# Two of a pair's 15 products exchange places, and the two chain banks exchange roles in every second pair

## The chip, the cores and the metric

One core of a Trainium2 chip runs the kernel. The metric is the device time of one execution in microseconds (us). An engine or queue is named as the profile names it: PE is TensorE's matmul, PEld its weight load, DVE is VectorE, ACT is ScalarE, POOL is GpSimd, SP is SyncE.

## The reference

A linear-attention recurrence over 768 steps for 2 x 8 heads of 48 gives x with 1536 rows and 384 columns. It then goes through four dense experts and a last gated layer:

```
p = domain_probs / (domain_probs.sum(-1) + 1e-9)
for e in range(4):                                   # w1[e] 384 x 1024, w2[e] 1024 x 384
    out += p[:, e:e+1] * (maximum(x @ w1[e], 0) @ w2[e])
h = out @ w_in                                       # 384 x 2048
y = (h * sigmoid(1.702 * h)) @ w_out                 # 2048 x 384
```

All of it is float32; the kernel splits every operand in a high and a low part and does three matmuls (high-high, high-low, low-high) where one product stands.

## The kernel before, in words

**Stages.** The attention and the first expert run first, mixed, up to about 150 us. Expert 1 to 3 and the gated layer then run as 20 "pairs" (numbered from 0): a pair is two tiles of 128 hidden columns each. Pair 12 (PLAIN), where the gated layer begins, is done in the plain way; the other 19 have both tiles against the 1536 rows, cut in three blocks of 512 rows, in the Strassen manner: 15 products on sums of weights and sums of rows in the place of 18.

**A product** (`product`, line 1946 in the profile) is three matmuls of 128x512 into one PSUM bank. The table PRODUCT (line 124) has its 15 rows in order: weight sum, rows, bank, whether it begins a new sum in its bank or goes on adding to what the bank holds, and then what is done with the bank: "copy" (ACT, `take`, line 1230) or "add" (DVE, `join`, lines 1570 and 1572) into result o, with a sign. The two banks, LEFT = 5 and RIGHT = 6, are the chain banks. A product waits until the copy or join of the product before it in the same bank has read the bank. In pair 0 some products use bank 3 or 4 instead (FIRST_BANKS, line 394): products 0, 12 and 13 use bank 3.

**A result** is one of six tiles: o = 3f + n, hidden tile f and row block n. The last product that goes into a result (LAST_OF) settles when it is complete, and DONE is the order in which the six get complete: place 0 is the first. By places, DVE gates the tile (`tile_gate`, line 1603), ACT copies its high part (`tile_high`, line 1248), and DVE takes its low part (`tile_low`, line 1613).

**A group** (`group`, line 1993) is six matmuls: the second weights of both hidden tiles against the tiles of row block n, three with f = 0 and three with f = 1, for output chunk k. A pair has nine, n in the order 1, 2, 0. The half for f waits until the low part of that tile is there. The groups of pair q stand on PE between the products of pair q + 1. A group's result is in bank 0 or 1, or by turns in banks 3 and 4 (SHARED); DVE adds it to the accumulator (`leave`, line 1585 or 1590). The very first group goes to bank 3, and so waits until pair 0's last use of bank 3 is over.

**The order** of each engine's work is a list made by `pairs`, and then, for some stretches, written out by hand (WRITTEN): p is a product, g a group, t a copy, j a join, m a gate, h a high part, l a low part, e a group's leaving; the number before the point is the pair. Each engine runs its list in that order. The stretch of DVE's list around the end of pair 0 reads

```
"... j0.10 j0.11 j0.12 m0.2 l0.0 j0.13 l0.1 l0.2 m0.3 j0.14 m0.4 j1.1 l0.3 m0.5 e0.1.0 j1.3 ..."
```

and PE's order there is p0.12, p0.13, p0.14, p1.0, g0.1.0 (the first group: pair 0, n = 1, k = 0), p1.1, p1.2, g0.1.1. Products of other pairs stand between groups, as in `p1.13 p1.14 g0.0.1 p2.0 g0.0.2 p2.1 p2.2`.

Of the kernel before, what the change touches and what calls it, by code (L numbers as in the profile page):

```python
# [122 lines left out]
LEFT, RIGHT = 5, 6  # L123
PRODUCT = (
    (2, (1, 0), LEFT, True, "copy", 0, 1),
    (10, (0, 0), LEFT, True, "add", 0, 1),
    (0, (1, 1), RIGHT, True, "copy", 1, 1),
    (12, 8, LEFT, False, "add", 1, -1),
    (9, 13, RIGHT, True, "copy", 4, 1),
    (7, 3, LEFT, False, "copy", 2, 1),  # L130
    (11, (2, 1), RIGHT, False, "add", 1, 1),
    (4, (0, 2), LEFT, False, "copy", 5, 1),
# [2 lines left out]
    (1, 4, LEFT, False, "add", 4, -1),  # L135
    (14, 10, RIGHT, False, "add", 5, -1),
    (6, (2, 2), LEFT, True, "add", 5, -1),
    (3, 1, LEFT, False, "add", 3, -1),
    (5, (1, 2), RIGHT, False, "add", 2, -1),
)  # L140

SUM_HOME = {13: 0, 8: 1, 14: 2, 3: 3, 9: 4, 1: 5, 10: (0, 1), 4: (2, 0)}
# [66 lines left out]
ADDED = [i for i, row in enumerate(PRODUCT) if row[4] == "add"]  # L209
# [5 lines left out]
def build(nc, rkT, rkvN, wu_rows, u_rows, weights, out):  # L215
    p_dram = nc.dram_tensor("p_normalised", [E, N], F32, kind="Internal").ap()
    ctx = ExitStack()
    with ctx:
# [10 lines left out]
        sem = {}  # L229
# [161 lines left out]

        OUT_SETS = ((7, 6, 5), (0, 1, 2))
        KEPT, SHARED, OVER = (0, 1), (3, 4), (2, 7)
        FIRST_BANKS = {0: SHARED[0], 2: SHARED[1], 12: SHARED[0], 13: SHARED[0]}
        PLAIN_BANKS, FIRST_OVER = (*OVER, LEFT, RIGHT), (OVER[1], SHARED[1], OVER[0], *KEPT, OVER[1])

        def out_tile(n, k):
# [125 lines left out]
        def kept_last(q):  # L523

            return q in (MOE_PAIRS - 1, ALL_PAIRS - 1)

        def kept_first(q):

            return q in (0, MOE_PAIRS)

        def kept(n, k):

            return n == 0 and k < len(KEPT)
# [6 lines left out]
        def wait_left(engine, q, n, k):  # L540

            if q == PLAIN:
                engine.wait_ge(sem["fresh"], THROUGH.index((n, k)) + 1)
            else:
                engine.wait_ge(sem["evac"], LEAVES[q, n, k] + 1)
# [5 lines left out]
        def place_of(q, f, n):  # L551

            return 2 * ROUND.index(n) + f if q == PLAIN else DONE.index(3 * f + n)
# [16 lines left out]

        def bank_of(q, i):

            return FIRST_BANKS.get(i, PRODUCT[i][2]) if q == 0 else PRODUCT[i][2]

        def result_of(q, pos):

# [12 lines left out]
        def shared_number(q, n, k):  # L589

            return len(THROUGH) * q + THROUGH.index((n, k))

        def shared_at(number):

            return (number // len(THROUGH), *THROUGH[number % len(THROUGH)])

        def shared_bank(q, n, k):

            return SHARED[shared_number(q, n, k) % len(SHARED)]
# [482 lines left out]
        def _(act):  # L1082
# [136 lines left out]
            def take(q, i):  # L1219

                _, _, _, _, _, o, sign = PRODUCT[i]
                number = t_number(q, o)
                act.wait_ge(sem["prod"], PRODS[q] + i + 1)
                if number >= T_RING:
                    act.wait_ge(sem["added"], t_before(number))
                    if q == 1:
                        act.wait_ge(sem["l2"], STEPS)
                elif t_tile(number) is t_of[number]:
                    act.wait_ge(sem["l2"], STEPS - 2)
                act.activation(t_tile(number), bank[:, bank_of(q, i), :], ACT.Copy, scale=float(sign)).then_inc(sem["copied"], 1)  # L1230
# [62 lines left out]
        def _(dve):  # L1293
# [252 lines left out]
            def join(q, i):  # L1546

                _, _, _, _, _, o, sign = PRODUCT[i]
                at = bank_of(q, i)
                t = t_tile(t_number(q, o))  # L1550
                before = [x for x in ADDED if x < i and PRODUCT[x][5] == o]
                dve.wait_ge(sem["prod"], PRODS[q] + i + 1)
                if before:
                    dve.wait_ge(sem["added"], JOINED[q] + ADDED.index(before[-1]) + 1)
                else:
                    dve.wait_ge(sem["copied"], TAKEN[q] + COPY_OF.index(o) + 1)
                new = t
                if LAST_OF[o] == i:
                    pos = DONE.index(o)
                    new = over_bank(q, pos)  # L1560
                    if q:
                        dve.wait_ge(sem["tlo"], 6 * q + pos - len(OVER) + 1)
                    elif pos == 1:
                        dve.wait_ge(sem["copied"], COPIED.index(2) + 1)
                    elif 1 < pos < 5:
                        dve.wait_ge(sem["ev1"], KT * len(SPANS))
                    elif pos == 5:
                        dve.wait_ge(sem["tlo"], 1)
                if sign > 0:
                    dve.tensor_tensor(new, bank[:, at, :], t, ALU.add).then_inc(sem["added"], 1)  # L1570
                else:
                    dve.scalar_tensor_tensor(new, bank[:, at, :], -1.0, t, ALU.mult, ALU.add).then_inc(sem["added"], 1)  # L1572
# [73 lines left out]
        def _(pe):  # L1646
# [275 lines left out]
            def product(q, i):  # L1922

                weight, rows, _, begins, _, _, _ = PRODUCT[i]
                at = bank_of(q, i)
                piece = next(n for n, (first, last) in enumerate(PIECES) if first <= weight < last)
                pe.wait_ge(sem["alo"], PARTS_W[q] + piece + 1)
                if q in (0, PLAIN + 1) and type(rows) is int:
                    pe.wait_ge(sem["slo"], len(SUM_ORDER) * (q > 0) + SUM_ORDER.index(rows) + 1)
                if q == PLAIN + 1 and i in (0, 2):  # L1930
                    pe.wait_ge(sem["tlo"], 6 * PLAIN + (3 if at == LEFT else 4))
                earlier = [x for x in range(i) if bank_of(q, x) == at]
                if earlier:
                    x, before = earlier[-1], q
                elif q and q != PLAIN + 1:
                    x, before = max(x for x in range(PRODUCTS) if bank_of(q - 1, x) == at), q - 1
                else:
                    x = None
                    if at in HID:
                        pe.wait_ge(sem["hlo"], STEPS - 1 + HID.index(at))  # L1940
                if x in COPIED:
                    pe.wait_ge(sem["copied"], TAKEN[before] + COPIED.index(x) + 1)
                elif x in ADDED:
                    pe.wait_ge(sem["added"], JOINED[before] + ADDED.index(x) + 1)
                for n, (a, c) in enumerate(PASSES):
                    last = pe.matmul(bank[:, at, :], a_parts[a][:, q % 2, weight * P:(weight + 1) * P], rows_of(ss[c], xs[c], rows),  # L1946
                                     start=(begins and n == 0), stop=(n == 2), skip_group_check=True)
                last.then_inc(sem["prod"], 1)
# [20 lines left out]
            def group(q, n, k):  # L1969

                begins, ends = (kept_first(q), kept_last(q)) if kept(n, k) else (True, True)
                if kept(n, k):
                    at = KEPT[k]
                    if q == 0:
                        pe.wait_ge(sem["ev1"], KT * len(SPANS))
                        pe.wait_ge(sem["tlo"], FIRST_OVER.index(at) + 1)
                    elif begins:
                        pe.wait_ge(sem["evac"], LEAVES[q - 1, n, k] + 1)
                else:
                    at = shared_bank(q, n, k)  # L1980
                    number = shared_number(q, n, k)
                    if number >= len(SHARED):
                        wait_left(pe, *shared_at(number - len(SHARED)))
                    elif number == 0:
                        pe.wait_ge(sem["added"], ADDED.index(13) + 1)
                    else:
                        pe.wait_ge(sem["tlo"], FIRST_OVER.index(at) + 1)
                pe.wait_ge(sem["vlo"], q + 1)
                for f in range(2):
                    number = 6 * q + place_of(q, f, n)  # L1990
                    pe.wait_ge(sem["tlo"], number + 1)
                    for i, (a, c) in enumerate(PASSES):
                        last = pe.matmul(bank[:, at, :], v_parts[a][q % 2][:, f * DM + k * P:f * DM + (k + 1) * P], tiles[c][number % H_RING],  # L1993
                                         start=(begins and f == 0 and i == 0), stop=(ends and f == 1 and i == 2))
                last.then_inc(sem["grp"], 1)
# [74 lines left out]
```

## Time and profile before

| | |
|---|---|
| median of 3 runs | 609.37 us (609.34 to 609.57) |
| the profiled execution | 609.61 us, span 607.6 us |
| PE busy | 598.9 us, 99% |
| DVE / ACT / POOL busy | 461.4 / 295.3 / 307.1 us |
| granted TensorE clock | 1.00 |

The time of an execution is that of its span and some 2 us around it. A row of a timeline gives start, duration, engine, line, operation, tiles out and in, and count; in brackets stands how long the engine had been idle and what released it. Matmuls are pipelined, so the duration of one (0.39 us) is longer than the distance between two starts (0.227 us); stalls are read from the starts.

### The profile page before, as it was taken

Reading aid. Unit: us, or ns where it says so; the run is one execution under the profiler, and the core shown is the slowest. Engines: PE = TensorE matmul, PEld = TensorE weight load, DVE = VectorE, ACT = ScalarE, POOL = GpSimd, SP = SyncE. Lnnn points to the kernel's source line nnn. Section 1 sums busy time; section 2 is a strip of 40 time slices with the busy share of each in tenths; the row PEclk is TensorE's granted clock in tenths of the full one; section 3 lists DMA queues with packets and bytes.
Section 4 is the critical chain, followed back from the end, with each engine's and each line's share of the span. In section 5 each row is a group of like instructions: output and inputs, shape, how many; then the busy total and the mean of one; then the engine's idle time right before and its main releaser. Section 6 shows DMA issues by size and latency. Waiting matters only on the chain.

```text
span 607.6 us, 10788 instructions
## 1 busy us (share of the span) xinstructions
PE 598.9 (99%) x3709; PEld 496.4 (82%) x3709; DVE 461.4 (76%) x752; ACT 295.3 (49%) x585; POOL 307.1 (51%) x369
## 2 busy tenths in 40 slices
PE   8999999989999999999999999999999999999997
PEld 5999988867688888888888888888887888888886
DVE  7888563454888877877877877788787887877895
ACT  4754533143544445345345335335776566556540
POOL 5654310599566455455446446326776745544200
PEclk9999999999999999999999999999999999999999
DMA  8766430001211110210010110100101110100004
GB/s 328 276 231 208 133 125 2 3 2 50 81 52 53 52 54 17 88 53 28 26 53 26 28 53 26 53 26 2 31 23 52 53 53 26 28 26 1 1 0 156
DMA packets 18171, 39.14 MB, mean 64 GB/s; under 512 B 1984, under 2 KB 9792, under 8 KB 18112
## 3 DMA queue, kind: packets, MB, share of 16 engines
q1 hardware_dynamic: 18112, 38.40, 18.8%
q8 instruction: 32, 0.52, 0.4%
q14 instruction: 27, 0.22, 0.1%
HBM read 36.01 MB, written 2.38 MB: 63 GB/s over the span
## 4 chain that ended last, share of the span: by engine, by line
PE 94%; DVE 2%; issue 1%; POOL 1%; DMA 1%; ACT 0%; SPq 0%; DVEq 0%; POOLq 0%; ACTq 0%
PE bank L1993 40%; PE bank L1946 32%; PE bank L1687 7%; PE bank L1712 7%; PE bank L1965 2%; PE bank L1746 2%; PE bank L1790 1%; PE bank L1793 1%; PE bank L1765 1%; PE bank L1780 1%; DMA rk_in<-rk_t 1%; PE bank L1783 0%; DVE s_lo L1538 0%; DVE acc L1623 0%; DVE bank L1572 0%
## 5 line engine op out<-in xcount | busy, mean ns | idle before, releaser
L1993 PE MATMUL bank<-w_lo,w_hi 128*128 128x512 f32 x729 | 186.1, 389 | 0.0
L1020 POOL TENSOR_TENSOR a_lo<-staging,a_hi 128x512 fp32r<-128x512 f32 (+3 forms) x96 | 97.7, 1026 | 146.9 <-ACT a_hi L1208 135.6
L1993 PEld LDWEIGHTS bank<-w_lo,w_hi 128*128 128x128 f32 x729 | 136.7, 188 | 29.0 <-DVE w_lo L1613 0.4
L1230 ACT ACTIVATE t_most<-bank 128x512 f32<-128x512 f32 x110 | 65.7, 598 | 55.7 <-PE bank L1946 54.9
L1993 PE MATMUL bank<-w_hi 128*128 128x512 f32 x351 | 91.8, 389 | 0.0
L1248 ACT ACTIVATE w_lo<-bank 128x512 fp32r<-128x512 f32 x81 | 48.0, 598 | 84.9 <-DVE bank L1603 52.9
L1585 DVE TENSOR_TENSOR acc<-bank,acc 128x512 f32<-128x512 f32 x86 | 58.7, 685 | 25.8 <-PE bank L1993 25.8
L1993 PEld LDWEIGHTS bank<-w_hi 128*128 128x128 f32 x351 | 65.9, 188 | 13.7
L1572 DVE SCALAR_TENSOR_TENSOR bank<-bank,t_most 128x512 f32<-128x512 f32 x92 | 63.9, 695 | 14.9 <-PE bank L1946 12.4
L1946 PE MATMUL bank<-x_hi,a_hi 128*128 128x512 f32 x171 | 66.6, 390 | 0.1
L1946 PE MATMUL bank<-x_lo,a_hi 128*128 128x512 f32 x171 | 66.5, 389 | 0.0
L1946 PE MATMUL bank<-x_hi,a_lo 128*128 128x512 f32 x171 | 66.5, 389 | 0.0
L1025 POOL TENSOR_TENSOR w_hi<-staging,w_hi 128x768 fp32r<-128x768 f32 x20 | 37.0, 1851 | 45.5 <-ACT w_hi L1217 45.5
L1613 DVE TENSOR_TENSOR w_lo<-bank,w_lo 128x512 fp32r<-128x512 f32 x81 | 55.3, 684 | 3.5 <-ACT w_lo L1248 1.2
L1208 ACT ACTIVATE a_hi<-staging 128x512 fp32r<-128x512 f32 (+2 forms) x95 | 48.0, 521 | 9.7 <-POOL staging L1061 5.7
L1946 PE MATMUL bank<-s_hi,a_hi 128*128 128x512 f32 x114 | 44.7, 392 | 1.6 <-DVE bank L1572 1.2
L1946 PE MATMUL bank<-s_lo,a_hi 128*128 128x512 f32 x114 | 44.4, 389 | 0.0
L1946 PE MATMUL bank<-s_hi,a_lo 128*128 128x512 f32 x114 | 44.4, 389 | 0.0
L1248 ACT ACTIVATE w_hi<-bank 128x512 fp32r<-128x512 f32 x39 | 23.3, 598 | 41.2 <-DVE bank L1603 26.6
L1109 ACT ACTIVATE h_hi<-bank 128x256 fp32r<-128x256 f32 (+1 forms) x32 | 15.6, 487 | 55.7 <-PE bank L1687 55.7
L1370 DVE SCALAR_TENSOR_TENSOR h_lo<-bank,h_hi 128x256 fp32r<-128x256 f32 (+1 forms) x32 | 17.6, 551 | 32.7 <-ACT h_hi L1109 32.6
L1946 PEld LDWEIGHTS bank<-x_hi,a_hi 128*128 128x128 f32 x171 | 32.1, 188 | 7.4 <-issue 0.5
(179 smaller groups left out, 1152.2 us busy)
## 6 DMA issues: line engine op xcount, KB each, us to landing
staging<-weights SPq DMA_DIRECT2D x40, 384.0 KB, 3.6
rkv_in<-rkv_n SPq DMA_DIRECT2D x10, 640.0 KB, 5.5
rk_in<-rk_t SPq DMA_DIRECT2D x12, 512.0 KB, 5.2
staging<-weights SPq DMA_DIRECT2D x4, 768.0 KB, 8.9
out<-acc SPq DMA_DIRECT2D x9, 256.0 KB, 2.0
p_bc<-p_normalised SPq DMA_DIRECT2D x2, 768.0 KB, 4.1
staging<-p_normalised SPq DMA_DIRECT2D x2, 768.0 KB, 5.6
rkv_in<-rkv_n SPq DMA_DIRECT2D x2, 448.0 KB, 5.8
```

What stands on the lines that cost most here:

```text
L1020: pool.tensor_tensor(new, src, high.bitcast(F32), ALU.subtract).then_inc(sem["alo"], 1)
L1025: pool.tensor_tensor(v_lo[q % 2], second_raw[q % 2], v_hi[q % 2].bitcast(F32), ALU.subtract).then_inc(sem["vlo"], 1)
L1208: act.activation(a_hi[:, q % 2, first * P:last * P].rearrange("p (i n) -> p i n", n=P), src, ACT.Copy).then_inc(sem["ahi"], 1)
L1230: act.activation(t_tile(number), bank[:, bank_of(q, i), :], ACT.Copy, scale=float(sign)).then_inc(sem["copied"], 1)
L1248: act.activation(tile_hi[number % H_RING], over_bank(q, pos), ACT.Copy).then_inc(sem["thi"], 1)
L1572: dve.scalar_tensor_tensor(new, bank[:, at, :], -1.0, t, ALU.mult, ALU.add).then_inc(sem["added"], 1)
L1585: dve.tensor_tensor(acc[:, k, cols], src, acc[:, k, cols], ALU.add).then_inc(sem["evac"], 1)
L1613: dve.tensor_tensor(tile_lo[number % H_RING], over_bank(q, pos), tile_hi[number % H_RING].bitcast(F32), ALU.subtract).then_inc(sem["tlo"], 1)
L1687: last = pe.matmul(bank[:, HID[j % 2], 0:tokens.stop - tokens.start], w[:, k, :], xs[c][:, k, tokens], start=(n == 0), stop=(n == 3 * KT - 1))
L1712: last = pe.matmul(out_tile(n, k), w[:, k * P:(k + 1) * P], hs[c][:, slot, 0:size],   start=(first and i == 0 and not (n < SMALLS and k == ...
L1946: last = pe.matmul(bank[:, at, :], a_parts[a][:, q % 2, weight * P:(weight + 1) * P], rows_of(ss[c], xs[c], rows), start=(begins and n == ...
L1993: last = pe.matmul(bank[:, at, :], v_parts[a][q % 2][:, f * DM + k * P:f * DM + (k + 1) * P], tiles[c][number % H_RING], start=(begins and ...
```

## The change

In PRODUCT the last two rows change places: product 13 is now the one in bank RIGHT that completes result 2, and product 14 the one in bank LEFT that completes result 3. DONE was 1, 0, 4, 5, 3, 2 and is now 1, 0, 4, 5, 2, 3. In pair 0, product 14 instead of 13 goes to bank 3, and the first group waits for the join of product 14 instead of 13. In pairs with an even number above 0, LEFT and RIGHT are exchanged. The lists of orders are as they were; they name products and results by their number and place.

```
@@ PRODUCT
     (6, (2, 2), LEFT, True, "add", 5, -1),
+    (5, (1, 2), RIGHT, False, "add", 2, -1),
     (3, 1, LEFT, False, "add", 3, -1),
-    (5, (1, 2), RIGHT, False, "add", 2, -1),
 )
@@ build
-        FIRST_BANKS = {0: SHARED[0], 2: SHARED[1], 12: SHARED[0], 13: SHARED[0]}
+        FIRST_BANKS = {0: SHARED[0], 2: SHARED[1], 12: SHARED[0], 14: SHARED[0]}
@@ bank_of
-            return FIRST_BANKS.get(i, PRODUCT[i][2]) if q == 0 else PRODUCT[i][2]
+            if q == 0:
+                return FIRST_BANKS.get(i, PRODUCT[i][2])
+
+            return LEFT + RIGHT - PRODUCT[i][2] if q % 2 == 0 else PRODUCT[i][2]
@@ group
                     elif number == 0:
-                        pe.wait_ge(sem["added"], ADDED.index(13) + 1)
+                        pe.wait_ge(sem["added"], ADDED.index(14) + 1)
```

## Rows read from the trace of the kernel before

**Rows 1.** The page: span, and PE's share of it.

```profile
span 607.6 us, 10788 instructions
...
PE 598.9 (99%) x3709; PEld 496.4 (82%) x3709; DVE 461.4 (76%) x752; ACT 295.3 (49%) x585; POOL 307.1 (51%) x369
```

**Rows 2.** Waits of PE on DVE at products: us in total, times, longest.

```profile
PE bank L1946 <- DVE bank L1572: 1.2, 2, 1.0
PE bank L1946 <- DVE t_rest L1570: 0.2, 1, 0.2
PE bank L1946 <- DVE t_most L1570: 0.2, 1, 0.2
```

**Rows 3.** The chain that ended last, its last three pieces (start, us, what).

```profile
588.07 16.33 PE bank L1993 x72
604.40 0.02 issue
604.43 0.69 DVE acc L1590
```

**Rows 4.** Timeline of PE from product 11 of pair 0 on.

```profile
159.10 0.39 PE L1946 MATMUL bank<-x_hi,a_lo 128*128 128x512 f32 x1
159.33 0.40 PE L1946 MATMUL bank<-x_hi,a_hi 128*128 128x512 f32 x1
...
161.15 0.47 PE L1946 MATMUL bank<-s_hi,a_hi 128*128 128x512 f32 x1 [0.98 <-DVE bank L1572]
...
161.92 0.39 PE L1946 MATMUL bank<-x_hi,a_hi 128*128 128x512 f32 x1
...
162.60 0.39 PE L1946 MATMUL bank<-x_hi,a_hi 128*128 128x512 f32 x1
...
163.28 1.74 PE L1993 MATMUL bank<-w_lo,w_hi 128*128 128x512 f32 x6
164.86 0.40 PE L1946 MATMUL bank<-x_hi,a_hi 128*128 128x512 f32 x1
```

**Rows 5.** Timeline of DVE in the same stretch.

```profile
159.53 0.69 DVE L1572 SCALAR_TENSOR_TENSOR part<-bank,part 128x512 f32<-128x512 f32 x1 [0.32 <-PE bank L1946]
160.31 0.70 DVE L1572 SCALAR_TENSOR_TENSOR bank<-bank,part 128x512 f32<-128x512 f32 x1
160.91 0.69 DVE L1603 SCALAR_TENSOR_TENSOR bank<-bank,staging 128x512 f32<-128x512 f32 x1
161.51 0.68 DVE L1613 TENSOR_TENSOR w_lo<-bank,w_lo 128x512 fp32r<-128x512 f32 x1
162.12 0.70 DVE L1572 SCALAR_TENSOR_TENSOR bank<-bank,t_most 128x512 f32<-128x512 f32 x1
162.72 1.28 DVE L1613 TENSOR_TENSOR w_lo<-bank,w_lo 128x512 fp32r<-128x512 f32 x2
163.92 0.69 DVE L1603 SCALAR_TENSOR_TENSOR bank<-bank,staging 128x512 f32<-128x512 f32 x1
164.52 0.69 DVE L1572 SCALAR_TENSOR_TENSOR bank<-bank,part 128x512 f32<-128x512 f32 x1
165.12 0.69 DVE L1603 SCALAR_TENSOR_TENSOR bank<-bank,staging 128x512 f32<-128x512 f32 x1
165.75 0.69 DVE L1570 TENSOR_TENSOR t_most<-bank,t_most 128x512 f32<-128x512 f32 x1
...
168.47 0.69 DVE L1572 SCALAR_TENSOR_TENSOR t_most<-bank,t_most 128x512 f32<-128x512 f32 x1 [0.24 <-PE bank L1946]
```

**Rows 6.** Weight loads of PE at the stalled product and in the first group.

```profile
161.12 0.19 PEld L1946 LDWEIGHTS bank<-s_hi,a_hi 128*128 128x128 f32 x1 [1.37 <-issue]
...
164.06 0.53 PEld L1993 LDWEIGHTS bank<-w_lo,w_hi 128*128 128x128 f32 x3 [0.36 <-DVE w_lo L1613]
```

**Rows 7.** Busy time by stretch: PE, PEld, DVE, ACT, POOL, granted clock, DMA share.

```profile
166.00:604.40 438.40, 438.19 (x1931) 361.77 (x1929) 352.25 (x547) 221.13 (x400) 219.94 (x272) 1.00 0.12 38
```

**Rows 8.** Timeline of PE at the start of the program.

```profile
1.39 3.59 PE L1650 MATMUL bank<-part 128*128 128x512 bf16 x8 [1.39 <-POOL part L846]
4.81 1.09 PE L1658 MATMUL bank<-ident,w_rev 128*128 128x128 f32 x4
5.69 0.86 PE L1650 MATMUL bank<-part 128*128 128x512 bf16 x2
6.63 1.16 PE L1746 MATMUL bank<-q_r_mid,q_k_mid 48*128 48x128 f32 x16
```

## The prediction

> **What bounds the kernel now.** I read the page first: PE is busy for 598.9 of 607.6 us [rows 1], so only what makes PE wait, or takes waits from it, can move the time. A busy PE may still hide small losses, because its matmul ends are modelled, so I turned to the waits. In the whole of the pairs PE waits for DVE at four places, 1.6 us in sum, and the longest is one of 1.0 us [rows 2]. From 166.00 to 604.40 us PE is busy for 438.19 of 438.40 us [rows 7]. The chain that ended last is groups without a break, then one DVE add [rows 3]. Its 72 matmuls give the pace of a PE that never waits: 16.33 / 72 = 0.2268 us from start to start, so a product costs 0.68 us and a group 1.36 us.
>
> How much could be hidden between? From the start of the first group at 163.28 [rows 4] to the end of the last matmul at 604.40 [rows 3] the program has 20 x 9 groups of 6, 18 pairs of 15 products of 3 less the 3 matmuls of the product that stands ahead of that group, and 6 x 9 plain ones: 1080 + 807 + 54 = 1941 matmuls. A matmul's end is 0.39 us after its start, so from first start to where the next would start there are 604.40 - 0.39 + 0.23 - 163.28 = 440.96 us; 1941 x 0.2268 = 440.2. About 0.7 us is lost in all of this, and two waits that can be named (0.22 us in the first group, below, and one of rows 2 with its restart, some 0.3) are most of it. Everything that the change loosens in pairs 1 to 19 is worth at most this 0.7 us.
>
> **Pairs 1 to 19: each wait that changes.** Product 13 now waits for the join of product 11 instead of that of 12, and product 14 for that of 12 instead of 11. The join of 12 was needed by product 13 and is now needed by the one behind it: looser by 0.68 us. Products 0 and 2 of the next pair waited for the joins of 13 and 14, in that order, and still do, because the exchange of LEFT and RIGHT in even pairs follows the exchange of the rows; without it product 0 would wait for the join of 14. The tiles: row block 2 needed places 3 and 5, now 3 and 4; row block 0 needed 1 and 4, now 1 and 5. Its groups are the last three of a pair, so the last tile has three groups (4.1 us) more. The copy into result 3's buffer in the next pair waits one join longer, but it is the sixth copy there, nine products on. A tile's high part waits for the last group of its ring slot's reader: at one place that is now the last group of the pair two before, which runs as the pair begins, while the high parts come in its second half. The same operations run in the same order on every engine, so there is no new instruction and no DMA is moved. Since PE hardly waits there, I cost all this at nothing. What covers it is PE's own queue, which is full; the end behind the last matmul [rows 3] is the same as well. The bound is a gain of 0.7 us.
>
> **The end of pair 0: this is where it is decided.** Here there are no groups between the products, and each wait shows. The rows read like this [rows 4]: product 11's last matmul starts at 159.10, product 12 at 159.33. Product 13 could start at 159.33 + 0.68 = 160.01, but it is in bank 3 like product 12 and waits for join 12, which DVE has from 160.31 to 161.01 [rows 5]; it starts at 161.15, 0.14 us behind the join's end. Product 14 starts at 161.92, product 0 of pair 1 at 162.60, the first group at 163.28, product 1 of pair 1 at 164.86. The group takes 164.86 - 163.28 = 1.58 us and not 1.36: its second half waits for the low part of place 2, the second of the two operations that end at 162.72 + 1.28 = 164.00, and its weights load at 164.06 [rows 6].
>
> Now with the change:
> - Product 13 goes to RIGHT and waits for join 11, which ends at 159.53 + 0.69 = 160.22. It starts at 160.22 + 0.14 = 160.36 instead of 161.15. It takes 0.77 us, as after every restart here (161.92 - 161.15), to 161.13.
> - Product 14 goes to bank 3 and waits for join 12: 161.01 + 0.14 = 161.15. Product 0 of pair 1 follows at 161.83, and PE is ready for the first group at 161.83 + 0.68 = 162.51. So far 0.77 us are won.
> - The first group uses bank 3 and must now wait for join 14. What is DVE doing? Its list has join 13, two low parts, a gate, and then join 14. In rows 5 those are 162.12, 162.72 (two), 163.92 and 164.52, and from 160.31 to 166.4 they follow each other without a pause, 0.60 us apart: DVE is backed up, so an earlier product doesn't bring any of them forward. Nothing ahead of them changes: joins 11 and 12 read products that start when they did, and the exchange of results changes only which buffer joins 13 and 14 read. Join 14 ends at 164.52 + 0.69 = 165.21.
> - The group starts at 165.21 + 0.14 = 165.35 instead of 163.28: 2.07 us later. The low part of place 2 has been there since 164.00, so the wait in the middle is gone. It takes 1.36 + 0.09 for the restart = 1.45 us, and product 1 of pair 1 starts at 166.80 instead of 164.86: **1.94 us later**.
> - Who is late next? Behind the waiting group on PE stands product 1 of pair 1, and join 1 of pair 1 waits for that. It started at 165.75 [rows 5], when DVE got to it; now DVE gets to it at the same time and waits until about 167.7, and what follows in its list (a low part, a gate, the leaving of the first group) is late by the same 1.9 us. They serve groups that are as late. DVE's first idle moment in before, 0.24 us at 168.47, shows that it follows PE again by then, so the ratio between the two is as before.
> - Is the delay made good later? PE has no pause that it could give up but the 0.5 us that remain in the bound above, and the operations behind these pauses are late together with PE. So it goes through to the end.
>
> Sum: 609.61 + 1.94 = 611.55 us for an execution like the profiled one; the median of before is 0.24 us lower: 609.37 + 1.94 = **611.3 us**, 0.32% slower.
>
> The unknown sizes: the restart and the semaphore (0.09 and 0.14 us) are each seen more than once, and an error is under 0.1. The bound of what the loosened waits give back is 0.7 us, so 610.6 at the low end. At the high end one more DVE operation (0.60 us) could come ahead of join 14, or the restarted group could need another restart: 612.0. I take the middle because each row of the sum is seen in the trace itself.
>
> **The rivals.**
>
> *The first group isn't held (no change).* If join 14 came straight after join 13 or the gate and low parts were quicker, so that it ended before 162.4 us, PE would run into the group at 162.51. Its second half would still wait for the low part of place 2, which DVE has at 164.00, and product 1 of pair 1 would start at 164.86 as before: 609.4 us. Against it speaks that DVE's order is fixed and rows 5 show it without a gap. I give this 7%.
>
> *The stall at product 13 is won and kept (faster).* This is the same with the low part of place 2 early as well: PE keeps the 0.77 us and the 0.22 us in the group: 609.37 - 0.99 = 608.4 us. It is decided by one thing, whether DVE has finished both the low part of place 2 and join 14 by some 163.1 us; in rows 5 they end at 164.00 and 165.21. 3%; even then the gain is 0.16%, under what can be told from no change.
>
> *The clock falls during the pause (slower still).* PE will be idle from the end of product 0 of pair 1 (161.83 + 2 x 0.23 + 0.39 = 162.7) to 165.35, 2.7 us. The waits of before in rows 2 are 1.0 us at most, so no row shows what a pause of 2.7 us does to the clock; the granted clock is 1.00 after all of them [rows 7]. What a low clock costs is seen at the start: eight matmuls of 512 columns start in 4.81 - 1.39 = 3.42 us, 0.43 us apiece, which is the pace of 1.2 GHz (although the clock's column says 1.00 there), and the slow stretch is over by 6.63 us [rows 8]. If PE went back to that state and needed as long to leave it, half of 6.63 - 1.39 = 5.2 us would be lost, 2.6 us: 613.9 us. The Trainium skill, "TensorE: Matmul & The Clock Gate", section "HAM oscillation — how this bites in real kernels", says that gaps in PE's work make the gate throttle it again, so that the work behind a gap starts at half rate. By that rule a single gap could bring this rival about; the trace neither shows nor excludes it. Since PE works without a pause both before and after this one gap, I give it 5%.
>
> **How the numbers follow.** The forecast has 85% (611.3 us), no change 7%, the kept gain 3%, the clock 5%. The measurement can tell about 0.2%, 1.2 us, from no change; the forecast's 1.94 us is above this, and its low end of 610.6 is right at it. Slower by over 0.2%: 85 + 5 less 2 for the forecast's low edge = 88%. Within 0.2%: 7 + 2 and most of the kept gain's 3, 10%. Faster: 2%, for a gain in the later pairs on top of the kept one. The range is that of the forecast, 610.6 to 612.0, wider by 0.2 us on each side for the distance between a profile and a median: 610.4 to 612.2 us. That leaves out the rivals, 15%.
>
> **What would show it.** In the trace after: product 13 of pair 0 starts near 160.4 and not 161.15, and the wait of 1.0 us at it shrinks to about 0.3. A new wait of PE (or of its weight load) on line 1993 for DVE line 1572 stands at about 162.5 to 165.3, 2.7 us long, and it is the longest in the pairs. On DVE the join at 162.12 reads the buffer `part` and the one at 164.52 `t_most`, the other way round than before. DVE gets an idle spell of nearly 2 us ahead of the join at about 167.7. All starts behind that are 1.9 us later, and the pace stays at 0.2268. I am wrong if DVE reaches join 14 sooner than 164.5, if new or vanished waits stand in pairs 1 to 19, or if starts are 0.43 us apart after the pause.

## The result, and the profile after

| | before | after |
|---|---|---|
| median | 609.47 us (609.34 to 609.91, 6 runs) | 613.0 us (611.47 to 613.35, 6 runs) |
| ratio | | 1.005, 95% interval 1.004 to 1.006 |
| the profiled execution | 609.61 us, span 607.6 us | 613.08 us, span 611.0 us |

The kernel became 0.5% slower. The forecast was 611.3 us, in a range of 610.4 to 612.2 us. The six executions took 611.47, 612.07, 612.92, 613.08, 613.12 and 613.35 us: two lie in the range, one of them at the forecast, and four lie above it. That spread, 1.9 us, is the first thing to see. The kernel before has 0.6 us here and 1.1 to 1.5 us in the larger batches below, where one of its 67 executions, at 1548.99 us, is left out; so the spread alone proves little, and the clock has to be read with it.

The page gives the new wait in its costliest group (before, then after). In the kernel before, groups had no idle time ahead of them:

```profile
L1993 PE MATMUL bank<-w_lo,w_hi 128*128 128x512 f32 x729 | 186.1, 389 | 0.0
```

```profile
L1996 PE MATMUL bank<-w_lo,w_hi 128*128 128x512 f32 x729 | 186.7, 391 | 2.5 <-DVE bank L1575 2.5
```

(All lines of the kernel after are 3 higher: products 1949, groups 1996, joins 1573 and 1575, gates 1606, low parts 1616.) The timeline of PE at the end of pair 0, against [rows 4]:

```profile
159.76 0.39 PE L1949 MATMUL bank<-x_hi,a_lo 128*128 128x512 f32 x1
160.33 0.47 PE L1949 MATMUL bank<-x_hi,a_hi 128*128 128x512 f32 x1 [0.18 <-DVE part L1575]
...
161.12 0.47 PE L1949 MATMUL bank<-s_hi,a_hi 128*128 128x512 f32 x1
...
161.89 0.39 PE L1949 MATMUL bank<-x_hi,a_hi 128*128 128x512 f32 x1
...
165.21 2.26 PE L1996 MATMUL bank<-w_lo,w_hi 128*128 128x512 f32 x6 [2.46 <-DVE bank L1575]
167.27 0.63 PE L1949 MATMUL bank<-x_hi,a_hi 128*128 128x512 f32 x1
167.70 0.63 PE L1949 MATMUL bank<-x_lo,a_hi 128*128 128x512 f32 x1
168.12 0.63 PE L1949 MATMUL bank<-x_hi,a_lo 128*128 128x512 f32 x1
...
169.66 1.55 PE L1996 MATMUL bank<-w_lo,w_hi 128*128 128x512 f32 x6
```

and that of DVE, against [rows 5]:

```profile
162.08 0.69 DVE L1575 SCALAR_TENSOR_TENSOR bank<-bank,part 128x512 f32<-128x512 f32 x1
162.68 1.28 DVE L1616 TENSOR_TENSOR w_lo<-bank,w_lo 128x512 fp32r<-128x512 f32 x2
163.87 0.69 DVE L1606 SCALAR_TENSOR_TENSOR bank<-bank,staging 128x512 f32<-128x512 f32 x1
164.47 0.69 DVE L1575 SCALAR_TENSOR_TENSOR bank<-bank,t_most 128x512 f32<-128x512 f32 x1
165.07 0.69 DVE L1606 SCALAR_TENSOR_TENSOR bank<-bank,staging 128x512 f32<-128x512 f32 x1
168.79 0.69 DVE L1573 TENSOR_TENSOR t_most<-bank,t_most 128x512 f32<-128x512 f32 x1 [3.03 <-PE bank L1949]
```

What to see. Up to the first group all is as forecast: product 13 at 160.33, product 14 at 161.12 without a stall, product 0 of pair 1 at 161.89, join 14 on `t_most` at 164.47 to 165.16, the group at 165.21. Then the forecast fails: matmuls start 0.43 us apart (167.27, 167.70, 168.12) instead of 0.227. The windows show why; the clock column stands ahead of the DMA share:

```profile
162.00:164.00 2.00, 0.75 (x4) 0.27 (x2) 2.00 (x5) 1.42 (x3) 0.00 (x0) 1.00 0.00 0
164.00:166.00 2.00, 0.79 (x3) 0.67 (x4) 1.76 (x3) 1.22 (x4) 1.18 (x2) 1.00 0.01 4
166.00:168.00 2.00, 2.00 (x6) 1.60 (x5) 0.00 (x0) 0.00 (x0) 1.93 (x3) 0.51 0.31 66
168.00:170.00 2.00, 2.00 (x7) 1.53 (x7) 1.21 (x3) 0.14 (x1) 2.00 (x3) 0.64 0.89 320
170.00:172.00 2.00, 2.00 (x11) 1.63 (x10) 1.35 (x4) 1.46 (x3) 1.33 (x2) 1.00 0.02 8
```

Behind the pause the granted clock is 0.51, that is 1.2 GHz of the two levels 1.2 and 2.4, and in the next 2 us it comes back. Six matmuls stand in a window that has ten or eleven at 2.4 GHz. Half-microsecond windows place the two edges:

```profile
165.50:166.00 0.50, 0.50 (x3) 0.39 (x3) 0.26 (x1) 0.00 (x0) 0.43 (x1) 1.00 0.00 0
166.00:166.50 0.50, 0.50 (x3) 0.39 (x2) 0.00 (x0) 0.00 (x0) 0.43 (x1) 0.52 0.00 0
169.00:169.50 0.50, 0.50 (x3) 0.40 (x2) 0.50 (x2) 0.00 (x0) 0.50 (x1) 0.57 1.07 426
169.50:170.00 0.50, 0.50 (x4) 0.41 (x3) 0.50 (x2) 0.14 (x1) 0.50 (x2) 1.00 0.60 240
```

The column still reads 1.00 all through the pause. It falls at about 166.0, some 0.8 us after the group has started, and is back at about 169.4. The group's own length says the same: six matmuls at 0.43 us would take 2.56 us, at 0.227 us 1.36 us, and it takes 167.27 - 165.21 = 2.06 us, so its first matmuls ran at full pace.

Measured from product 12's last matmul (159.79 before, 159.76 after), the second group starts 166.23 - 159.79 = 6.44 us later in the kernel before and 169.66 - 159.76 = 9.90 us later in this one: 3.46 us lost at one place. The two parts can be told apart here. The group starts 5.45 us behind that matmul instead of 3.49, 1.96 us late; had it then taken the forecast 1.45 us instead of the 1.58 us of before, the loss would be 1.83 us, and the other 1.63 us are the slow matmuls. Nothing is lost or won behind it. The chain after has the same last stretch, 72 matmuls in 16.33 us as in [rows 3], and ends 3.46 us later:

```profile
591.53 16.33 PE bank L1996 x72
607.86 0.02 issue
607.88 0.69 DVE acc L1593
```

But those windows show a second thing that happens at the same time: the DMA share is 0.89 where the matmuls are slow. The traces already speak against the transfers as the cause. The matmuls are slow from 166.0 us on, while the share is still 0.00, and the kernel before has the same burst under matmuls at full clock:

```profile
168.00:170.00 2.00, 2.00 (x10) 1.65 (x10) 1.75 (x4) 1.97 (x4) 2.00 (x2) 1.00 0.91 305
```

Experiment 1 tries it in the changed kernel.

### The profile page after: what moved, and what is told of

Its sections match the earlier page's. It is cut to its first block, busy times and chain, and to the rows that moved or that the text cites. A ratio compares the mean times of both kernels' runs of the same rounds, so it can differ in the third digit from the quotient of the medians.

```text
span 611.0 us, 10788 instructions
## 1 busy us (share of the span) xinstructions
PE 600.4 (98%) x3709; PEld 497.7 (81%) x3709; DVE 461.3 (76%) x752; ACT 295.3 (48%) x585; POOL 307.4 (50%) x369
## 4 chain that ended last, share of the span: by engine, by line
PE 93%; DVE 3%; issue 2%; POOL 1%; DMA 0%; ACT 0%; DVEq 0%; POOLq 0%; ACTq 0%
PE bank L1996 40%; PE bank L1949 31%; PE bank L1690 7%; PE bank L1715 7%; PE bank L1968 2%; PE bank L1749 2%; PE bank L1793 1%; PE bank L1796 1%; PE bank L1783 1%; PE bank L1768 1%; PE bank L1786 0%; DMA wu_sb<-wu_rows 0%; DVE s_lo L1541 0%; DVE bank L1575 0%; DVE w_pow L1301 0%
```

## The experiments

They were run in three batches, each on another chip and each beside the kernel before on the same chip. Experiments 1 to 4 are the first batch and 5a, 6, 7a and 7b the second, both with a median of 609.66 us for the kernel before; 5b, 5c and 5d are the third, with 609.58 us. The mean granted clock of an execution is 1.000 or 0.999 where nothing fell (the kernel before has both). Theory A: the wait for join 14 costs 1.9 us, and the pause that it makes lets the clock fall, which costs the rest. Theory B: the rest comes from the transfers. Theory C: it comes from the later pairs.

**1. The pause filled with work** (added to the kernel after).

```
                     product(q, *rest)
+                    if (q, *rest) == (1, 0):
+                        pe.wait_ge(sem["added"], ADDED.index(13) + 1)
+                        for _ in range(9):
+                            pe.matmul(bank[:, RIGHT, :], a_parts[0][:, 1, 2 * P:3 * P], xs[0][:, 1, 0:NB], start=True, stop=True, ...)
```

> The changed kernel with nine extra matmuls, whose result nobody reads, in bank 6 between product 0 of pair 1 and the first group. Theory A (the wait for join 14 costs 1.9 us, and the rest of the loss is TensorE's clock, which fell because of the pause): the group starts when it did, near 165.2, the pause shrinks from 2.6 to under 0.5 us, the granted clock stays at 1.00, and the time is 611.3 us in every execution, without the spread of 611.5 to 613.4. Theory B (the rest of the loss comes from elsewhere, as a burst of DMA that slows the matmuls behind the group): matmuls behind the group still start 0.43 us apart for some 4 us, and the time stays near 613.0.

Measured: 611.53 us (611.27 to 611.83, 5 runs), ratio 1.0034 (1.0021 to 1.0047). PE's timeline and its windows:

```profile
162.72 2.32 PE L2008 MATMUL bank<-x_hi,a_hi 128*128 128x512 f32 x9
165.11 1.66 PE L1996 MATMUL bank<-w_lo,w_hi 128*128 128x512 f32 x6
166.60 0.39 PE L1949 MATMUL bank<-x_hi,a_hi 128*128 128x512 f32 x1
```

```profile
165.20:167.00 1.80, 1.80 (x8) 1.49 (x9) 0.45 (x1) 0.08 (x1) 1.50 (x3) 1.00 0.00 0
167.00:169.00 2.00, 2.00 (x10) 1.65 (x10) 1.51 (x3) 0.83 (x2) 2.00 (x3) 1.00 0.83 252
```

Nine useless matmuls make the kernel some 1.5 us faster (611.53 against 613.0 us, and against 612.93 us in experiment 4 of the same batch). The group starts no sooner (165.11), but the clock stays at 1.00, the spread is 0.6 us, and the same burst of transfers (share 0.83) passes under matmuls at full pace. Theory B is out.

**2. The wait alone**, in the kernel before: `ADDED.index(13) + 1` becomes `ADDED.index(14) + 1`, and nothing else changes.

> The kernel before with one wait lengthened: the first group waits for the join of product 14 instead of 13. No row of PRODUCT and no bank is exchanged. Theory A: join 14 ends at 165.2 as in both kernels, so the group starts at 165.35 and product 1 of pair 1 at 166.8, 1.94 us late; the pause in front of the group is 2.07 less 0.2 us, a fifth shorter than the 2.6 us of the changed kernel, so the clock falls as often or less often: 611.4 us where it does not fall, up to 613.4 where it does. Theory C (the later pairs' exchange is what costs the rest): 611.4 us in every execution, granted clock 1.00.

Measured: 611.33, 611.35, 612.18, 613.22 and 613.24 us, ratio 1.004 (1.0027 to 1.0053). PE waits 1.8 us at the first group, and in the profiled execution (613.24 us) the windows 165.20 to 167.00 and 167.00 to 169.00 have a clock of 0.73 and 0.50. The lengthened wait alone brings both parts of the loss.

**3. The change in pairs 1 to 19 alone.** The table, the order of completion and the banks depend on the pair (cut, against the kernel after):

```
+EXCHANGED = (*PRODUCT[:13], PRODUCT[14], PRODUCT[13])
+def rows_in(q):
+    return EXCHANGED if q == 0 else PRODUCT
...
-        FIRST_BANKS = {0: SHARED[0], 2: SHARED[1], 12: SHARED[0], 14: SHARED[0]}
+        FIRST_BANKS = {0: SHARED[0], 2: SHARED[1], 12: SHARED[0], 13: SHARED[0]}
```

and the first group waits for join 13.

> The change in pairs 1 to 19 alone: pair 0 has its rows, its banks and its wait as before. Theory A: the looser waits of the later pairs give nothing and cost nothing: 609.4 us, within 0.3, PE starts its first group at 163.3 with the 1.0 us stall at product 13 back. Theory C: the later pairs cost 1.7 us: 611.1 us. The bound of a gain is 0.7 us: 608.8.

Measured: 609.38 us (609.14 to 610.5, 11 runs), ratio 1.0000 (0.9991 to 1.0009). PE's waits in the pairs are those of before, the 1.0 us at product 13 among them. Theory C is out, and the looser waits of 18 pairs give nothing that can be told (the interval is 0.5 us to either side).

**4. The change in pair 0 alone**: `EXCHANGED` and `PRODUCT` the other way round, no exchange of banks in even pairs.

> The change in pair 0 alone: the later pairs keep their rows and banks. Theory A: the whole of the loss, with its spread: 611.4 to 613.4 us, median 613.0, group at 165.2, clock down for 4 us behind it in most executions. Theory C: 611.3 us, no spread.

Measured: 612.93 us (611.68 to 613.8, 6 runs), ratio 1.0051 (1.0039 to 1.0063): two executions at 611.7, four from 612.8 to 613.8. It is the whole of the change's effect, with its spread. That this run would have no fall under theory C was badly put; the pause is in pair 0 under any theory, so it tells only where the loss is.

**5. How the clock depends on the pause.** Join 14 is moved in DVE's list, in the kernel after; the rest of the list is as it was.

```
 after:  ... j0.13 l0.1 l0.2 m0.3 j0.14 m0.4 j1.1 l0.3 m0.5 ...
 5a:     ... j0.13 j0.14 l0.1 l0.2 m0.3 m0.4 j1.1 l0.3 m0.5 ...
 5b:     ... j0.13 l0.1 j0.14 l0.2 m0.3 m0.4 j1.1 l0.3 m0.5 ...
 5c:     ... j0.13 l0.1 l0.2 j0.14 m0.3 m0.4 j1.1 l0.3 m0.5 ...
 5d:     ... j0.13 l0.1 l0.2 m0.3 m0.4 l0.3 j0.14 j1.1 m0.5 ...
```

5a: 

> The changed kernel with join 14 of pair 0 moved on DVE to stand right behind join 13, ahead of two low parts and a gate. Theory A: join 14 ends near 163.4 instead of 165.2, the group starts at 163.5 after a pause of 0.9 us, its second half waits for the low part of place 2, now 0.6 us later (164.6), and product 1 of pair 1 starts near 165.4: 0.6 us later than in the kernel before, the clock stays at 1.00, so 610.0 us in every execution. If a pause of 0.9 us were enough to lower the clock: 611.7.

5b: 

> The changed kernel with join 14 of pair 0 on DVE between the low parts of places 1 and 2. The pause in front of the first group shrinks from 2.5 to 1.3 us (join 14 ends at 164.0). Without any fall of the clock product 1 of pair 1 starts 0.75 us later than in the kernel before: 610.3 us. Theory A with falls more frequent the longer the pause: none or few, since waits of 1.0 us in the kernel before and 1.4 us in the run with gate 2 early left the clock at 1.00: 610.3, spread under 1 us. If the clock fell: 612.1.

5c: 

> The same with join 14 behind both low parts and ahead of the gate of place 3: a pause of 1.9 us. Without a fall 1.35 us later than before: 610.9 us; with one 612.8. Theory A: some executions at each level, as with the lengthened wait of the kernel before, whose pause was 1.8 us and whose five times were 611.3, 611.4, 612.2, 613.2, 613.2.

5d: 

> The same with join 14 behind two more operations of DVE (gate of place 4, low part of place 3): a pause of 3.7 us. Without a fall 3.15 us later than before: 612.7 us. Theory A: the clock falls in every execution, 614.5 us or a little more, with little spread. If falls did not depend on the pause's length, the two levels 612.7 and 614.6 would be mixed as in the changed kernel.

The table has all kernels with this wait; 5b, 5c and 5d share one chip.

| kernel | wait of PE at the first group | median | ratio (interval) | executions with a clock of 0.997 or less |
|---|---|---|---|---|
| 1, pause filled | none listed | 611.53 | 1.0034 (1.0021 to 1.0047) | 0 of 5 |
| 5a | 0.7 and 0.2 us | 609.89 | 1.0007 (0.9998 to 1.0016) | 0 of 11 |
| 5b | 1.3 us | 610.11 | 1.0011 (1.0002 to 1.0019) | 0 of 11 |
| 2, wait alone | 1.8 us | 612.18 | 1.004 (1.0027 to 1.0053) | 2 of 5 |
| 5c | 1.9 us | 611.02 | 1.0035 (1.0021 to 1.0049) | 2 of 6 |
| the kernel after | 2.5 us | 613.0 | 1.005 (1.004 to 1.006) | 4 of 6 |
| 4, pair 0 alone | 2.5 us | 612.93 | 1.0051 (1.0039 to 1.0063) | 4 of 6 |
| 5d | 3.8 us | 614.61 | 1.0088 (1.0075 to 1.0101) | 5 of 5 |

The two levels stand out in 5c: 610.61, 610.75, 610.87 and 611.17 us with a clock of 1.00, 612.79 and 613.05 us with 0.997, where 610.9 and 612.8 were expected. PE's line at the first group in 5c's profiled execution, which kept its clock, and then in 5d's, which did not:

```profile
164.70 1.66 PE L1996 MATMUL bank<-w_lo,w_hi 128*128 128x512 f32 x6 [1.87 <-DVE bank L1575]
```

```profile
166.80 2.48 PE L1996 MATMUL bank<-w_lo,w_hi 128*128 128x512 f32 x6 [3.85 <-DVE bank L1575]
```

The join's place sets the length of the pause one DVE operation at a time, and the pause's length goes with how often the clock falls: in none of the 22 executions with waits of 0.7 and 1.3 us, in 4 of 11 with 1.8 and 1.9 us, in 8 of 12 with 2.5 us, in all 5 with 3.8 us. The ends of this row are clear of each other; its neighbouring steps (4 of 11 against 8 of 12) are too few executions to be told apart. The chip of 5b, 5c and 5d alone gives the same row: 0 of 11, 2 of 6, 5 of 5. For one and the same kernel it is decided anew in every execution.

Two executions lie between the levels, 612.07 us in the kernel after (mean clock 1.000) and 612.18 us in experiment 2 (0.999). Their clocks don't show a fall, and as only one execution of each kernel was traced, their times stay unexplained. So does the longest of 5d, 616.01 us with a clock of 0.994.

Four profiled executions had a fall. The edges in this table are estimates, worked out from the mean clock of windows of 0.5 and 1 us (0.52 in 166.00 to 166.50 means that it fell at 166.02):

| kernel | pause | group starts | clock falls | clock is back |
|---|---|---|---|---|
| 2 | 1.8 us | 165.40 | 166.0 | 169.4 |
| the kernel after | 2.5 us | 165.21 | 166.0 | 169.4 |
| 4 | 2.5 us | 164.99 | 165.4 | 168.8 |
| 5d | 3.8 us | 166.80 | 167.4 | 170.8 |

All four look alike: the column reads 1.00 through the pause, falls 0.4 to 0.8 us after the group has started, and is back some 3.4 us later. So with a longer pause falls were more frequent, but not longer.

**6. Other work ahead of the waiting group**: in PE's list of the kernel after, `p1.0 p1.1 p1.2 g0.1.0 g0.1.1` instead of `p1.0 g0.1.0 p1.1 p1.2 g0.1.1`.

> The changed kernel with products 1 and 2 of pair 1 put ahead of the first group on PE. DVE is as in the changed kernel, so join 14 still ends at 165.2. Product 1 waits for the copy of product 0 (ACT, ends near 163.3) and starts at 163.4, product 2 at 164.2, the group at 165.3, the second group at 166.8 instead of 166.2 in the kernel before. Theory A: 0.6 us slower than before, 610.0 us, clock at 1.00, because the one pause of 2.6 us has become two short ones with work between.

Measured: 610.2 us (609.8 to 610.59, 11 runs), ratio 1.0008 (0.9999 to 1.0017). Join 14 comes no earlier, but PE works meanwhile; its longest wait there is 0.8 us, for ACT's copy of product 0, and the clock fell in none of the 11.

**7. Two attempts to beat the kernel before.** 7a is the kernel after with DVE's list as `j0.10 m0.2 j0.11 j0.12 l0.0 j0.13 j0.14 l0.2 l0.1 m0.3 m0.4`; 7b is the kernel before with `j0.10 m0.2 j0.11 j0.12 l0.0 l0.2 j0.13 l0.1 m0.3 j0.14 m0.4`.

7a: 

> The changed kernel with DVE's list around the end of pair 0 set for the new wait: gate 2 ahead of join 11 (it falls into DVE's idle 0.3 us), join 14 right behind join 13, the low part of place 2 ahead of that of place 1. Join 14 ends near 163.0, the low part of place 2 near 163.6, product 1 of pair 1 starts near 164.5 instead of 164.86 in the kernel before: 609.0 to 609.2 us, 0.3 us under the kernel before, which is less than can be told; clock 1.00.

7b: 

> The kernel before with gate 2 ahead of join 11 on DVE and the low part of place 2 ahead of join 13. The 1.0 us stall at product 13 stays (join 12 isn't earlier), the wait of 0.22 us in the middle of the first group goes: 609.2 us, 0.2 us under the kernel before.

Measured: 609.95 us (609.56 to 610.56, 11 runs), ratio 1.0005 (0.9996 to 1.0014), and 609.67 us (609.35 to 610.15, 11 runs), ratio 1.0001 (0.9992 to 1.001). Neither wins. The clock fell in neither, though 7b has a stall of 1.4 us at product 13. DVE's timeline of 7a shows why:

```profile
158.65 0.70 DVE L1575 SCALAR_TENSOR_TENSOR bank<-bank,t_most 128x512 f32<-128x512 f32 x1
159.46 0.70 DVE L1606 SCALAR_TENSOR_TENSOR bank<-bank,staging 128x512 f32<-128x512 f32 x1
160.06 0.68 DVE L1575 SCALAR_TENSOR_TENSOR part<-bank,part 128x512 f32<-128x512 f32 x1
```

The gate (1606) waits for what the join ahead of it writes, so it starts at 159.46, 0.81 us behind the join's start and not 0.6. It does not fit in DVE's idle 0.3 us, join 11 comes later, and product 13 waits 0.57 us instead of 0.18. [Rows 5] had this already: join 12 adds to what join 11 wrote, and starts 160.31 - 159.53 = 0.78 us behind it.

7a has a second reason. Join 14 ended at 163.35 and the group started at 163.41, but its second half waited again:

```profile
163.26 1.28 DVE L1616 TENSOR_TENSOR w_lo<-bank,w_lo 128x512 fp32r<-128x512 f32 x2
164.59 0.96 PE L1996 MATMUL bank<-w_lo,w_hi 128*128 128x512 f32 x3 [0.22 <-DVE w_lo L1616]
```

The half waits with `pe.wait_ge(sem["tlo"], number + 1)`, that is until three low parts are done, whichever they are. With the low part of place 2 ahead of that of place 1, three are still done only at 163.26 + 1.28 = 164.54, so the exchange of the two gave nothing, and product 1 of pair 1 starts at 165.39 instead of the expected 164.5. In 7b the stall at product 13 grew from 0.98 to 1.36 us by the gate, and product 1 of pair 1 starts 165.14 - 159.87 = 5.27 us behind product 12's last matmul instead of 5.07: more than the 0.22 us was lost again.

## Why the prediction was wrong

**Right.** The end of pair 0 decides; pairs 1 to 19 are worth nothing (experiment 3, within 0.09%). Product 13 was forecast for 160.36 and starts at 160.33, product 14 for 161.15 and starts at 161.12. Join 14 cannot be brought forward because DVE's list is backed up: it ends at 165.16, forecast 165.21. The group was forecast for 165.35 and starts at 165.21, so the gap between join and group is 0.05 to 0.14 us. The delay of 1.94 us is about what executions show whose clock does not fall, each against its own kernel before: 2.0 us in the kernel after (611.47), 1.7 us in experiment 2 (611.33 and 611.35), 2.0 us in experiment 4 (611.68 and 611.72) and 1.87 us in experiment 1 (611.53). The delay goes through to the end.

**Wrong.** The step that failed is the clock. The sum has it at nothing, and the only reason is in the rival: "Since PE works without a pause both before and after this one gap, I give it 5%." No row bears on that sentence. The new wait would leave PE idle for 2.7 us by the prediction's own working, and the trace of before has no such pause behind work at full clock. Its longest is 1.42 us, in the first expert, and the clock is 1.00 before and behind it:

```profile
131.40 0.50 PE L1687 MATMUL bank<-x_hi,w_hi 128*128 128x512 f32 x1 [1.42 <-DVE h_lo L1370]
```

The prediction took 1.0 us, from the pairs alone [rows 2]; neither length could speak for or against 2.7 us. In the runs the clock fell in 4 of 6 executions, and in 4 of 6 again in experiment 4, so this rival was the likeliest case, and the median of 613.0 us is the forecast's delay plus a fall. The Trainium skill, "TensorE: Matmul & The Clock Gate", section "HAM oscillation — how this bites in real kernels", says that waits of some 3 to 5 us for DMA get PE throttled, so that the next stretch of work starts cold. The prediction cites it as "gaps", without their length. The windows of the kernel after agree for a shorter gap, of 2.5 us (0.51 behind it), and so does experiment 2 for 1.8 us; 5a and 5b show gaps of 0.7 and 1.3 us that don't do it.

The price of that rival was too high: 2.6 us, from the start of the program, where the slow stretch runs from 1.39 to 6.63 us [rows 8]. Measured, the levels with and without a fall are 613.1 - 611.5 = 1.6 us apart in the kernel after, 613.2 - 611.3 = 1.9 us in experiment 2, 1.5 us in experiment 4 and 2.1 us in 5c. The group takes 2.06 us instead of the forecast 1.45, and the clock is back at about 169.4. The chances have a slip too: 7 + 2 and most of 3 is 11% and not 10%, which changes nothing.

The last line of the prediction named starts 0.43 us apart as what would make it wrong, and that is what came.

## What to carry to other kernels

Where TensorE is busy all the time, price a new wait twice: for its length, and for what its length does to the clock behind it. If the trace has no pause of that length at full clock, an execution at each level has to be reckoned with, and a forecast needs both. A wait on a semaphore of an engine with a written order costs what stands ahead of the signalling operation in that order: here one place in DVE's list is 0.6 us. Where a wait is for a count, moving one of the counted operations ahead of another gains nothing (7a). If the wait can't be had shorter, put other matmuls in front of it, useful ones (experiment 6), for even useless ones paid (experiment 1).

## What the runs showed of the hardware that was not expected

- One kernel has two levels of time, 1.5 to 2.1 us apart, by whether TensorE's clock falls behind a single pause of 1.8 to 2.5 us; at 1.3 us it fell in none of 11 executions, at 3.8 us in all of 5.
- The clock column reads 1.00 all through the pause; the fall comes 0.4 to 0.8 us after the work has begun again, in all four traces that have one. The low stretch is some 3.4 us long in all four, for pauses of 1.8 to 3.8 us.
- The clock averaged over the run shows a fall as 0.997 against 1.000, easily taken for nothing.
- A burst of transfers (share 0.83, 252 GB/s in experiment 1; share 0.91, 305 GB/s in the kernel before) left the pace of the matmuls at full clock unchanged.
- A DVE operation that waits for what the one ahead of it writes starts 0.81 us behind that one's start (158.65 to 159.46; 0.78 us in [rows 5]), an independent one 0.60 us behind (159.46 to 160.06).
